# Attention groups of a fused kernel in pairs: scores beside the earlier pair's values, turns in a block of their own

## What is computed

```python
# q, k, v: (4 batches, 8 heads, 576, 64); heads 0-3 local mask (32 keys back), heads 4-7 strided (every 32nd)
attn = softmax(mask(q @ k.T / 8)); o = attn @ v
x = o as (2304 tokens, 512)
xn = x / sqrt(mean(x * x) + 1e-6) * rms_g
x = (silu(xn @ w_gate) * (xn @ w_val)) @ w_out          # d_ff 1536
e = argmax(x @ router + bias[modality]); g = softmax(...)[e]
out = g * (relu(x @ w1[e]) @ w2[e])                      # 8 experts, d_ff 1024
```

## Time and profile before

| what | value |
|---|---|
| time, median of 3 runs | 868.03 us (867.34 to 871.87) |
| profiled execution, its own time | 867.06 us |
| its span, first to last instruction | 865.3 us |
| mean granted share of TensorE's clock | 0.999 |
| busy: PE, DVE, ACT, POOL | 98%, 60%, 44%, 38% |
| from the first score of group 28 to the last values | 141.9 to 375.4 us |

### The profile page before, as it was taken

One profiled execution on the slowest core, in us unless ns is written; L12 is line 12 of the kernel. 1 busy time (PEld: TensorE's weight loads), 2 busy tenths in 40 slices (PEclk: granted clock), 3 DMA queues, 4 the chain that ended last, 5 costly groups with the idle time before them and its releaser, 6 DMA issues.

```text
span 865.3 us, 15529 instructions
## 1 busy us (share of the span) xinstructions
PE 852.3 (98%) x5194; PEld 728.4 (84%) x5203; DVE 522.9 (60%) x1400; ACT 376.7 (44%) x948; POOL 332.3 (38%) x373
## 2 busy tenths in 40 slices
PE   8999999999999999999999999999999999999997
PEld 5678898888888888899999998987888888888885
DVE  5985555333453335549778773883877456666664
ACT  5967413545454454543231132143455235554442
POOL 3736762344333443247336433170043221222212
PEclk9999999999999999999999999999999999999999
DMA  9983212222114210241221121527265645555531
GB/s 191 284 201 108 61 49 66 72 68 78 52 46 116 65 37 26 73 158 50 60 99 61 49 85 37 206 87 256 98 206 204 245 143 189 187 216 182 189 132 46
DMA packets 77517, 103.40 MB, mean 119 GB/s; under 512 B 38973, under 2 KB 43069, under 8 KB 77312
## 3 DMA queue, kind: packets, MB, share of 16 engines
q1 hardware_dynamic: 73760, 91.16, 34.1%
q0 software_dynamic: 3680, 11.28, 3.7%
HBM read 92.98 MB, written 10.22 MB: 119 GB/s over the span
## 4 chain that ended last, share of the span: by engine, by line
PE 89%; DVE 8%; issue 1%; ACT 1%; POOL 1%; DVEq 0%; ACTq 0%; POOLq 0%
PE ps L1229 32%; PE ps L1268 16%; PE ps L1812 13%; PE ps L1797 13%; PE ps L1160 3%; PE ps L1189 2%; PE ps L1170 2%; PE ps L1822 2%; PE ps L1137 2%; PE ps L658 1%; PE ps L1310 1%; DVE sm L1523 1%; DVE w_lo L2051 1%; DVE h_lo L1603 1%; DVE w_lo L861 1%
## 5 line engine op out<-in xcount | busy, mean ns | idle before, releaser
L1034 POOL TENSOR_TENSOR sm<-sm,rinv 72x288 f32<-72x288 f32 (+1 forms) x51 | 45.6, 894 | 174.1 <-DVE rinv L1534 174.1
L1066 POOL TENSOR_TENSOR out_lo<-out_raw,out_hi 128x512 fp32r<-128x512 f32 x72 | 102.7, 1426 | 5.8
L1064 POOL CAST out_hi<-out_raw 128x512 fp32r<-128x512 f32 x72 | 52.0, 723 | 128.8 <-DMA out_raw<-in_moe_w_out 128.8
L1592 DVE SCALAR_TENSOR_TENSOR h<-h,ps 128x384 f32<-128x384 f32 x72 | 39.8, 553 | 102.0 <-ACT h L1430 101.0
L1229 PE MATMUL ps<-x_hi,val_hi 128*128 128x384 f32 x288 | 100.8, 350 | 0.0
L1229 PE MATMUL ps<-x_hi,gate_hi 128*128 128x384 f32 x288 | 100.3, 348 | 0.4 <-DVE h L1592 0.4
L1229 PE MATMUL ps<-x_hi,gate_lo 128*128 128x384 f32 x288 | 96.8, 336 | 0.0
L1229 PE MATMUL ps<-x_hi,val_lo 128*128 128x384 f32 x288 | 96.5, 335 | 0.0
L1229 PE MATMUL ps<-x_lo,val_hi 128*128 128x384 f32 x288 | 96.4, 335 | 0.0
L1434 ACT ACTIVATE h_hi<-h 128x384 fp32r<-128x384 f32 x72 | 37.9, 527 | 134.3 <-DVE h L1598 134.3
L1229 PE MATMUL ps<-x_lo,gate_hi 128*128 128x384 f32 x288 | 93.6, 335 | 0.0
(11 more groups left out here) (287 smaller groups left out, 1938.0 us busy)
## 6 DMA issues: line engine op xcount, KB each, us to landing
w_raw<-in_moe_w SPq DMA_DIRECT2D x72, 512.0 KB, 3.5
out_raw<-in_moe_w_out SPq DMA_DIRECT2D x72, 256.0 KB, 2.6
x_rows<-y_tiles SPq DMA_DIRECT2D x18, 256.0 KB, 2.7
early_w_raw<-in_moe_w SPq DMA_DIRECT2D x8, 512.0 KB, 3.5
gate_raw<-in_moe_w_gate SPq DMA_DIRECT2D x4, 768.0 KB, 8.4
val_raw<-in_moe_w_val SPq DMA_DIRECT2D x4, 768.0 KB, 10.4
qk<-in_q SPq DMA_DIRECT2D x8, 288.0 KB
qk<-in_k SPq DMA_DIRECT2D x8, 288.0 KB
```

The costliest lines, as they stand in the source:

```text
L1034: pool.tensor_tensor(s3, s3, rinv[0:n, i, :].unsqueeze(2).to_broadcast([n, 4, c]), ALU.mult).then_inc(s_no, 1)
L1064: pool.tensor_copy(oh[i][:, :], o_raw[i][:, :]).then_inc(s_oh, 1)
L1066: pool.tensor_tensor(ol[i][:, :], o_raw[i][:, :], oh[i][:, :].bitcast(f32), ALU.subtract).then_inc(s_ol, 1)
L1592: dve.scalar_tensor_tensor(out=hf[n % 2][:, :], in0=hf[n % 2][:, :], scalar=1.0, in1=ps[:, 0, 0:CH], op0=ALU.add, op1=ALU.mult).then_inc(s ...
```

## The change

From group 28 on two neighbouring groups are one pair, and a pair comes every twelve ticks. Both are scored at the same tick (86, 98, ..., 242), the odd one in the other half of the same two banks. Both are turned ten ticks later, before the down product, into banks 5 and 6. Their values come two ticks after that, behind the scores of the next pair and in two halves of bank 7, and one ACT instruction evacuates both. The later two q/k tiles are turned six ticks ahead of the scores and no longer three. The mask of a pair waits for both scores; the scores of a pair wait for the evacuation of the turned probabilities of the pair before.

```diff
-    return EARLY + SPAN - 6 + 6 * (j - 2 * NG)
+    return EARLY + SPAN - 6 + 12 * ((j - 2 * NG) // 2)
...
-TURN = {j: SCORE[j] + (3 if j < HEAD - 3 else 7 if j < 2 * NG else 6) for j in range(G)}
+PAIRS = 2 * NG
+TURN = {j: SCORE[j] + (3 if j < HEAD - 3 else 7 if j < PAIRS else 10) for j in range(G)}
 TURN.update({HEAD - 3 + i: EARLY + 1 + 2 * i for i in range(3)})
-PV = {j: TURN[j] + (1 if j < HEAD - 1 else 2 if j < 2 * NG else 3) for j in range(G)}
+PV = {j: TURN[j] + (1 if j < HEAD - 1 else 2) for j in range(G)}
...
+for j in range(PAIRS, G):
+    EXPS[j], INVERT[j], NORM[j] = (SCORE[j] + x + j % 2 * y for x, y in ((1, 1), (4, 2), (5, 2)))
...
-    return [s - 7, s - 5, s - 4, s - 2] if b < 2 else [s - 9, s - 9, s - 3, s - 3]
+    return [s - 7, s - 5, s - 4, s - 2] if b < 2 else [s - 9, s - 9, s - 6, s - 6]
...
 BANK7 = [x for s in range(TICKS) for x in
-         [("p", j) for j in TURN_AT.get(s, [])] + [("o", j) for j in PV_AT.get(s, []) if s >= EARLY]
+         [("p", j) for j in TURN_AT.get(s, []) if j < PAIRS]
+         + [("o", j) for j in PV_AT.get(s, []) if s >= EARLY and (j < PAIRS or j % 2 == 0)]
...
+        def p_bank(j):
+            return 7 if j < PAIRS else 5 + j % 2
+
+        def pair_col(j):
+            return 256 * (j % 2) if j >= PAIRS else 0
...
                     scores_read(s)
+                    pe.wait_ge(s_pe, TURNED_PROBS[s])
...
                 if j:
-                    pe.wait_ge(s_m, 4 * j)
+                    pe.wait_ge(s_m, 4 * (j if j < PAIRS else j - j % 2))
+                if j >= PAIRS:
+                    pe.wait_ge(s_pe, j - j % 2)
...
-                bank_7_free(("p", j))
+                if j < PAIRS:
+                    bank_7_free(("p", j))
+                else:
+                    scores_read(TURN[j])
+                    pe.wait_ge(s_qe, TURNED_QK[TURN[j]])
...
                 if s >= EARLY:
-                    bank_7_free(("o", j))
+                    if j < PAIRS or j % 2 == 0:
+                        bank_7_free(("o", j))
...
+            def evac_o_pair(j):
...
+                act.wait_ge(s_pv, j + 2)
+                if j % NG == 0:
+                    act.wait_ge(s_xl, KT * b)
...
+                act.activation(dst, src, ACT.Copy).then_inc(s_oe, 2)
...
                 for j in PV_AT.get(s, []):
-                    evac_o(j)
+                    if j < PAIRS:
+                        evac_o(j)
+                    elif j % 2 == 0:
+                        evac_o_pair(j)
...
-                dve.wait_ge(s_s, j + 1)
+                dve.wait_ge(s_s, j + 1 if j < PAIRS else j - j % 2 + 2)
```

More of the change, by code:

```diff
@@ L109 @@
 VALUED = [sum(x < s for x in PV.values()) for s in range(TICKS + 1)]
+TURNED_PROBS = [sum(x < s for x in TURN.values()) for s in range(TICKS + 1)]
 TURNED_QK = [sum(x < s for x in QK.values()) for s in range(TICKS + 1)]
@@ L1100, in bank_7_free @@
                 elif before[0] == "o":
-                    pe.wait_ge(s_oe, before[1] + 1)
+                    pe.wait_ge(s_oe, before[1] + (1 if before[1] < PAIRS else 2))
                 elif before[0] == "ss":
@@ L1158, in score @@
                         lhs, rhs = qT[hp % 2][hs, x:x + SQ], kT[hp % 2][hs, WIN + x:WIN + x + SQ]
-                    mm = pe.matmul(ps[0:n, bank + i // 2, (i % 2) * c:(i % 2 + 1) * c], lhs, rhs,
+                    at_col = pair_col(j) + i % 2 * c
+                    mm = pe.matmul(ps[0:n, bank + i // 2, at_col:at_col + c], lhs, rhs,
                                    start=True, stop=True)
@@ L1166, in turn_probs @@
                 n, c = rows(hp), keys(hp)
-                bank_7_free(("p", j))
+                if j < PAIRS:
[3 more added lines that the diff above has]
+                    pe.wait_ge(s_qe, TURNED_QK[TURN[j]])
                 pe.wait_ge(s_no, j + 1)
                 for i in range(4):
-                    mm = pe.transpose(ps[0:c, 7, i * n:(i + 1) * n], sm[PLACE[j]][0:n, i * c:(i + 1) * c],
+                    mm = pe.transpose(ps[0:c, p_bank(j), i * n:(i + 1) * n], sm[PLACE[j]][0:n, i * c:(i + 1) * c],
                                       ident[0:n, 0:n])
@@ L1188, in values @@
                     vals = vloc[hp][:, h, u, :] if is_loc(hp) else vstr[hp - 2][:, h, u * D:(u + 1) * D]
-                    mm = pe.matmul(ps[64 * h:64 * h + 64, bank, (u % 2) * n:(u % 2 + 1) * n], vals,
+                    at_col = pair_col(j) + u % 2 * n
+                    mm = pe.matmul(ps[64 * h:64 * h + 64, bank, at_col:at_col + n], vals,
                                    pt[j % 2][0:c, i * n:(i + 1) * n], start=True, stop=True)
@@ L1390, in evac_probs @@
                     act.wait_ge(s_pv, j - 1)
-                act.activation(pt[j % 2][0:c, 0:4 * n], ps[0:c, 7, 0:4 * n], ACT.Copy).then_inc(s_pe, 1)
+                act.activation(pt[j % 2][0:c, 0:4 * n], ps[0:c, p_bank(j), 0:4 * n], ACT.Copy).then_inc(s_pe, 1)
             def evac_o(j):
@@ L1397, in evac_o @@
                 act.wait_ge(s_pv, j + 1)
-                if b >= 2 and j % NG == 0:
-                    act.wait_ge(s_xl, KT * b)
                 src = ps[:, o_bank(j), 0:2 * n]
@@ L1407, in evac_o @@
                 act.activation(dst, src, ACT.Copy).then_inc(s_oe, 1)
+            def evac_o_pair(j):
+                b, hp, g = place(j)
+                n = rows(hp)
+                act.wait_ge(s_pv, j + 2)
+                if j % NG == 0:
+                    act.wait_ge(s_xl, KT * b)
+                src = ps[:, 7, :].rearrange("d (a x) -> d a x", a=2)[:, :, 0:2 * n]
+                if not is_loc(hp):
+                    dst = xT[:, hp, b % 2 * S:b % 2 * S + S].rearrange("d (p r) -> d r p", r=SU)
+                    dst = dst[:, 2 * g:2 * g + 4, :].rearrange("d (a r) p -> d a r p", a=2)
+                    src = src.rearrange("d a (r p) -> d a r p", p=n)
+                elif place(j + 1)[1] == hp:
+                    dst = xT[:, hp, b % 2 * S + 2 * g * n:b % 2 * S + (2 * g + 4) * n]
+                    dst = dst.rearrange("d (a x) -> d a x", a=2)
+                else:
+                    dst = xT[:, hp:hp + 2, b % 2 * S + 2 * g * n:b % 2 * S + (2 * g + 2) * n]
+                act.activation(dst, src, ACT.Copy).then_inc(s_oe, 2)
             def exps(j):
@@ L1523, in mask_max @@
                     dve.tensor_tensor_reduce(out=sm[k_][0:n, i * c:(i + 1) * c],
-                                             in0=ps[0:n, bank + i // 2, (i % 2) * c:(i % 2 + 1) * c], in1=mask,
+                                             in0=ps[0:n, bank + i // 2, pair_col(j) + i % 2 * c:
+                                                    pair_col(j) + (i % 2 + 1) * c], in1=mask,
                                              scale=-float(D) ** -0.5, scalar=3.0e38, op0=ALU.add, op1=ALU.min,
```

## The result

The changed kernel takes 862.65 us (median of 5 runs, 862.40 to 865.16), the kernel before in the same session 868.67 (5 runs). The ratio is 0.9941, 95% interval 0.9923 to 0.9958: 5.1 us faster by the ratio, 6.0 by the medians, where the prediction's sum was 9.9. The time lies inside the range on record but outside the 856.5 to 860 that was forecast as likely, and about half of the forecast gain is missing.

What follows compares the result with a forecast made beforehand. PE's own stream of records was taken as the bound; -11.5 + 0.1 + 0.7 - 0.2 + 0.9 + 0.1 = -9.9 us gave 857.2 profiled, 858.1 median. Likely 856.5 to 860 (0.68), range 856 to 863.5.

Steps and rivals of the forecast that it cites:

- Prices of blocks: PE's attention blocks: pairing saves 0.81 us per 72-row pair and 0.84 per 96-row pair, 11.5 us over 14 pairs.
- 11.5 - 0.1 - 0.7 = 10.7: Gain on PE's blocks, less 0.1 us for lone first scores and last values and 0.7 for q/k tiles turned alone.
- Both rivals about PE: Two slower cases for PE's paired blocks, each giving 862.7 us; chances 0.17 and 0.06.
- a loss at the second group: In PE's paired blocks, the second group of a kind loses as much as the first; +4.6 us, 862.7; chance 0.17.
- records without lead: PE's records run out of lead in a pair's block of 32 short records; 4.6 us, 862.7; chance 0.06.
- h_lo at chunk ends: POOL's normalising goes first and delays h_lo on DVE; PE waits 0.3, 0.7 and 0.7 us at three chunk ends, +0.9.
- The wait of the pair's scores for `s_pe` has behind it everything on PE ... nine down matmuls are 2.07: Scores waiting for ACT's evacuation of turned probabilities: covered by down matmuls, 0.8 us to spare, else the excess 13 times.
- On POOL the second normalising ... I get 1.3 us to spare: POOL normalises a pair's second group before its turns with 1.3 us to spare; only tick 140 adds, +0.1.
- turns wait for POOL: PE's turn of a pair's second group waits for late POOL, 14 times; 872.5 us at 2.3 late; chance 0.03.
- The case that happened, waits at pairs: Partial loss on PE: small waits of 0.2 to 0.4 us at each pair, 860 to 863.5 us; chance 0.06.
- One sign of being wrong: Wrong if the stretch from the first pair's scores to the last values isn't shorter by 8 us or more.
- POOL's sm was to show at most once: Sign in PE's waits after the change: h_lo at three places, POOL's sm at most once.

Runs made afterwards that it cites:

- the kernel with all remedies: Kernel after, with turns earlier, inverse and normalising early but behind h_lo at chunk ends, and roots spread a tick later; 858.82 us, ratio 0.9894.
- the alternating ones: Blocks of the kernel after reordered to scores, values, scores, values instead of two and two; 866.89 us, ratio 0.9982.

## Why the prediction was half right

**Prices of blocks: right, some 0.8 us too good.** All attention blocks of the stretch, by the prediction's measure (with the usual distances of two products, 0.173 and 0.232 us), add up to 52.0 us before and 42.1 in the kernel with all remedies: 9.9 less, where 11.5 - 0.1 - 0.7 = 10.7 had been worked out. About 0.5 of the difference lies in the kernel before: its scores, turns and values make 45.2 us, by the prediction's prices 45.7, each of which is too high by about 0.01. Another 0.1 are q/k tiles, which behind values had cost 0.47 to 0.50 and not 0.52. The rest is 96-row groups after: scores and values of 96 rows 2.19, not 2.08 (four), with one kind of 96 rows 0.06 more than the pieces (three), against turns of 96 rows at 0.70, not 0.76 (six). The timeline after shows 40 attention blocks, not 45; before there are 57, not 59, and after, three of the turns touch the scores behind them.

**Both rivals about PE: wrong.** Neither a loss at the second group nor records without lead: 16 scores in 0.73 us and 16 values in 0.65 (72 rows), where a loss at the second group would have shown 0.84 and 0.82. The Trainium skill, TensorEngine Tiling (Array Packing), § Key Properties, has the drain at a change of tiling mode and none at a change of tile; the blocks here and the alternating ones agree, at 0.11 to 0.13 us a change.

**h_lo at chunk ends: right.** 0.34, 0.71 and 0.71 against 0.3, 0.7 and 0.7, by the mechanism named; putting the inverse behind it took them away.

**"The wait of the pair's scores for `s_pe` has behind it everything on PE ... nine down matmuls are 2.07": this step failed**, at 3 of 13 places. It was worked out for a step in the middle of a chunk and multiplied by 13. In a chunk's first step the nine matmuls aren't there, and the excess that the step itself named comes due: 2.3 us. Had each of the 13 ticks been looked up, it would have stood in the sum.

**"On POOL the second normalising ... I get 1.3 us to spare": this step failed** at ticks 144, 156 and 228. It went through POOL's own queue and left out when the odd group's inverse leaves DVE. At ticks 156 and 228 that stands behind the roots, which the first normalising, by moving a split into them, makes longer. At tick 144 POOL's queue was seen, but its cost was put at 0.1 and was 0.4. Together 2.1 us instead of 0.1; with the inverse and the normalising early and the roots spread later, no wait for sm is left and these turns cost 0.70. This is the "turns wait for POOL" rival in kind, at 3 turns and not at 14, and so not slower than before.

**The sum again with what was measured:** -9.9 for blocks, -0.2 where turns and roots touch, -0.2 where turns and scores touch, +2.3, +2.1, and +0.8 for h_lo (+0.9 forecast) make -5.1; the stretch shows -4.9. That 862.65 nearly equals the 862.7 of two rivals is chance: their mechanisms are absent. The case that happened, waits at pairs, had been given 0.06 and was thought of as many small ones.

**One sign of being wrong didn't tell.** From the first pair's scores to the end of the last values it is 8.0 us less (233.7 before, 225.7 after), which just meets the 8 that were asked for. But the last values now stand at tick 254 and no longer at 257, ahead of 18 product matmuls, 3.1 us, that lay inside that stretch before; without them it is the 4.9 again. The waits told more: POOL's sm was to show at most once, and shows three times.

## What to carry to other kernels

When a wait is costed at nothing because other work covers it, list every place where it occurs and check the cover at each one, above all at the first and last step of a loop, where a term is left out. Follow a new wait back through the engine that feeds the one named: its inputs have a queue too. And moving work from one engine's queue can slow another that it shares a lock with; here it paid to keep POOL away from h_lo, and to give the roots six down matmuls more, rather than to make everything early.

## What was unexpected of the hardware

- Steps of 128x3 on DVE, 0.16 us alone, take up to 1.15 beside POOL, since they end only 0.01 to 0.03 us behind the instruction that POOL has under way. From the variance to the diagonals the chain of the roots takes 2.36 us before, 3.55 in the kernel after and 5.61 with the inverse early.
- It isn't only for instructions with two tensors: the integer step on `variance` alone took 0.39 us at 230.49 in the kernel after and ended, at 230.88, with POOL's cast (230.85). The cast itself took 0.94 us there, behind h_lo, against 0.61 alone: either engine holds up the other.
- Between groups of one kind PE loses nothing with 72 rows (and at most 0.05 us with 96), though each group has its own semaphore waits; each change of shape inside a block costs 0.11 to 0.13 us.
